# One kernel on one NeuronCore: the running sum of the kept counts and one low part of a weight piece stand behind the first expert's row blocks on VectorE

## The chip, the cores and the metric

The kernel runs on one core of one Trainium2 chip. A core has five engines that run their own instruction streams and wait for each other by semaphores: TensorE (PE; its weight loads are shown as PEld), VectorE (DVE), ScalarE (ACT), GpSimd (POOL) and SyncE (SP, which here only issues DMAs). The metric is the device time of one execution in microseconds, from the first to the last instruction and what lies around them; the median of the runs counts.

## The reference, cut to what matters

Three stages follow each other: a linear attention with a complex decay (its state is a running product, which the kernel computes in chunks), a mixture of experts in which each of 1536 tokens goes to one of 8 experts with room for 384 each, and a bilinear layer.

```python
def _moe_ref(x, w_gate, w1, w2, capacity):
    logits = x @ w_gate
    expert_idx = np.argmax(logits, axis=1)
    ...
    for i in range(N):
        e = expert_idx[i]
        if counts[e] < capacity:
            disp[e, counts[e]] = x[i]
            pos[i] = counts[e]
            counts[e] += 1
            keep[i] = True
    h = np.maximum(np.einsum('ecd,edf->ecf', disp, w1), 0.0)
    y = np.einsum('ecf,efd->ecd', h, w2)
    ...
            out[i] = gate_w[i] * y[expert_idx[i], pos[i]]

def _moe2_ref(x, w_a, w_b, w_out):
    return (x @ w_a) * (x @ w_b) @ w_out
```

The sizes: D = 384, F = 1024, so an expert has NF = 8 column blocks of 128 and KC = 3 row blocks of 128.

## The kernel before, in words

The attention is computed in chunks of 96 tokens for all heads; the gate's logits come out with it, and each chunk's rows are scattered by GpSimd to the place of their expert in a buffer in HBM (`sorted_x`, L795). The last chunks' rows of the first expert don't go through HBM: they are added by matmuls with a 0/1 matrix into three PSUM banks (`rows_bank`, L824). After the last chunk one matmul gives the number of tokens of each expert on all partitions (L979).

Every product with a weight is made exact enough by three matmuls: a value is split into a high part (`..h`, a copy on ACT into the matmul's reduced type) and a low part (`..l`, value minus high part, on DVE). `split` (L1008) issues this pair. For the first expert there are 8 such pieces of w1 (`piece1`, from `queries`, where the first w1 was loaded early), 3 row blocks (`xh`, `xl`, from PSUM) and 8 pieces of w2.

Between the chunks and the experts stands the code that the change touches (L1037 to L1050). DVE clips the counts to the capacity (`kept`, L1039), forms their running sum (`cumk`, L1040) and from it where each expert's first column lies in the output (`fst`, L1041), and casts both to integers (`first`, L1042, `nkept`, L1043). `kept`, `cumk`, `fst` and `one8` are the four slices of one tile, `total`, of 128 x 8 x 4 floats. Then come three weight pieces, the three row blocks and the five other weight pieces.

`nkept` is read by PE (L1117): each expert's matmuls exist for 224 and for 384 columns, and its count picks one. `first` is read by ACT and DVE (L1174, L1175) when they store an expert's outputs at their columns of `yh` and `yl`. POOL clears these two with memsets of 128 x 4608 (L1076) when the last scatter has landed.

`hidden` (L1115) makes the first product of an expert, `outputs` (L1171) the second. In `hidden`, PE takes column blocks f = 0 to 7, each of 9 matmuls (L1129), into four PSUM banks in turn; for the first expert f = 0 and 1 are interleaved by row block. From f = 4 on PE waits until block f - 4 has been read from its bank, that is, for `hl` (L1165) of that block. On ACT and DVE the blocks' `hh` (L1163) and `hl` alternate with w2's pieces. Each engine runs its instructions in the order in which the code issues them. SP loads the next w1 when DVE has made the eighth low part of w1 (L1055). A loop over the six middle experts follows, then the last one, then the bilinear stage in three tiles of 512 tokens.

Of the kernel before, what the change touches and what calls it, by code (L numbers as in the profile page):

```python
# [24 lines left out]
ALU = mybir.AluOpType  # L25
ACT = mybir.ActivationFunctionType
# [42 lines left out]
def build(nc, dims, qk, v, vt, a, w_gate, w1, w2, wa, wb, wo, out, CAP):  # L69
# [12 lines left out]
    KC = DM // P  # L82
    E = w_gate.shape[1]
    F = w1.shape[2]
    NF = F // P
# [14 lines left out]
    def sem(name):  # L100
        return ctx.enter_context(nc.semaphore(name))

    with ctx:
        pe, dve, act, pool = (Queue(nc, n, sem(f"s_{n}")) for n in ("pe", "dve", "act", "pool"))
        sp = nc.sync

        def sb(name, shape, dt=F32, at=ctx, side="left"):
            return at.enter_context(nc.sbuf_tensor(name, shape, dt, side=side))
# [16 lines left out]
        first = sb("first", [P, E], I32)  # L125
        nkept = sb("nkept", [P, E], I32)
# [33 lines left out]
        with att:  # L160
# [83 lines left out]
            vv, ss = nc.vector, nc.scalar  # L244
            tt, stt = vv.tensor_tensor, vv.scalar_tensor_tensor
# [432 lines left out]
            m_oh, m_slot, m_rk, m_tk, m_so, m_hot, m_part_x, m_read_lg = ({} for _ in range(8))  # L678
            s_row0 = sem("s_row0")
            LATE = TAU - 2  # L680
            rows_bank = [bank[i] for i in (2, 3, 6)]
# [300 lines left out]
            kept, cumk, fst, one8 = (total[:, :, i] for i in range(4))  # L982
            pe_chunks, dve_chunks = pe.n, dve.n

            def D_(ins):
                dve.wait(dve.done(ins))
                return (dve, dve.n, False)
# [7 lines left out]
            xh, xl = (sb(n_, [P, KC, CAP], F32R, at=exp_r, side="right") for n_ in ("xh", "xl"))  # L995
# [9 lines left out]
            def z32(x):  # L1005
                return x.bitcast(F32)

            def split(dst_h, dst_l, src):  # L1008

                m = act.done(ss.activation(dst_h, src, ACT.Copy))  # L1010
                dve.wait(m)
                return dve.done(tt(dst_l, src, z32(dst_h), ALU.subtract))  # L1012

            def piece1(f, at_first=False):
                src = raw_0[0].rearrange("p (c f) -> p c f", c=KC) if at_first else raw1
                return [x[:, :, f * P:(f + 1) * P] for x in (w1h, w1l, src)]
# [15 lines left out]
            pe_done, dve_done = (pe, pe_chunks, False), (dve, dve_chunks, False)  # L1032
# [3 lines left out]
            m_w1, m_x0 = [], []  # L1036
            dve.done(vv.memset(one8, 1.0))  # L1037
            dve.wait(m_tl)
            D_(vv.tensor_scalar(kept, rk, float(CAP), None, ALU.min))  # L1039
            D_(vv.tensor_tensor_scan(out=cumk, data0=one8, data1=kept, initial=0.0, op0=ALU.mult, op1=ALU.add))  # L1040
            D_(tt(fst, cumk, kept, ALU.subtract))  # L1041
            dve.done(vv.tensor_copy(first[:], fst))  # L1042
            m_first = dve.done(vv.tensor_copy(nkept[:], kept))  # L1043
            for f in range(NF):
                m_w1.append(split(*piece1(f, True)))
                if f == 2:
                    for c in range(KC):
                        act.wait(m_part_x[c])
                        m_x0.append(split(xh[:, c, :], xl[:, c, :], rows_bank[c][:, 0:CAP]))
                    act.wait(pe_done, dve_done)  # L1050
            sp.wait_ge(pe.sem, pe_chunks)
            sp.wait_ge(dve.sem, dve_chunks)
            sp.wait_ge(s_sc, 16 * TAU)
# [41 lines left out]
            return dve.done(tt(xl[:, :, i * P:(i + 1) * P], s_, z32(xh[:, :, i * P:(i + 1) * P]), ALU.subtract))  # L1095


        pe.wait(m_first)
        PART = 224
        assert PART <= (XT_N - 1) * P  # L1100
        ENG = [mybir.EngineType.PE, mybir.EngineType.DVE, mybir.EngineType.Activation, mybir.EngineType.SP]
# [210 lines left out]
        kept, fst = total[:, :, 0], total[:, :, 2]  # L1312
# [173 lines left out]
```

## Time and profile before

| | us |
|---|---|
| median of 3 runs | 579.62 |
| lowest and highest | 579.06, 599.04 |
| the profiled execution | 581.07 |
| its span, first to last instruction | 579.8 |
| PE busy | 536.5 (93%) |
| DVE busy | 369.1 (64%) |
| ACT busy | 292.6 (50%) |
| POOL busy | 50.8 (9%) |
| mean granted clock of TensorE | 0.969 |

Times in the views are microseconds from the start of the span. A row of the timeline gives start, length, engine, line, operation, what is written and read, and how many instructions of one kind follow each other; the brackets tell how long the engine had stood idle and what released it. Consecutive instructions of one engine overlap a little: a low part of a 128 x 384 piece lasts 0.55 us, while the next starts 0.47 us after it. The matmuls' ends are modelled. A PE busy share of 93% is not PE at its peak.

### The profile page before, as it was taken

What the parts mean: (1) busy time and instruction counts of PE and PEld (TensorE: products, weight loads), DVE (VectorE), ACT (ScalarE), POOL (GpSimd) and SP (SyncE); (2) the same over time, 40 slices, a digit from 0 to 9 for tenths busy, and PEclk for the clock granted to TensorE, in tenths of its full rate; (3) what the DMA queues carried; (4) which work ended last, traced back from release to release, by engine and by line L of the source; (5) the groups of instructions that cost most, each with busy time, mean ns of one, the idle gap of its engine ahead of it and who ended that gap; (6) DMA issues with size and microseconds to landing.
All of it is one profiled execution on the core that took longest, in us unless ns stands there. A gap on an engine that the chain in (4) does not pass through costs nothing.

```text
span 579.8 us, 10188 instructions
## 1 busy us (share of the span) xinstructions
PE 536.5 (93%) x3735; PEld 478.6 (83%) x3736; DVE 369.1 (64%) x900; ACT 292.6 (50%) x681; POOL 50.8 (9%) x63
## 2 busy tenths in 40 slices
PE   0499697889999989999999999999999999999996
PEld 0277365589999989999999998888888888888886
DVE  5998999979889898988888876453321221122121
ACT  5656448656556577878777764443231121311212
POOL 1000000001121233000000000430020000200002
PEclk9967699999999999999999999999999999999999
DMA  8999012589423137656776649720010000100001
GB/s 323 274 388 344 8 54 111 164 230 309 107 63 93 34 112 226 233 191 238 258 252 195 230 137 67 159 83 0 0 55 1 0 1 0 57 0 1 0 1 54
DMA packets 46321, 73.27 MB, mean 126 GB/s; under 512 B 16520, under 2 KB 38792, under 8 KB 45384
## 3 DMA queue, kind: packets, MB, share of 16 engines
q1 hardware_dynamic: 44360, 67.97, 38.5%
q0 software_dynamic: 1920, 4.75, 2.6%
q8 instruction: 27, 0.44, 0.3%
q14 instruction: 14, 0.11, 0.1%
HBM read 55.76 MB, written 16.97 MB: 125 GB/s over the span
## 4 chain that ended last, share of the span: by engine, by line
PE 80%; DVE 9%; ACT 5%; DMA 4%; issue 1%; POOL 0%; SPq 0%; DVEq 0%; POOLq 0%; ACTq 0%
PE psum L1380 26%; PE psum L1353 12%; PE psum L1186 11%; PE psum L1129 11%; PE psum L906 4%; DMA region<-x_rows 3%; PE psum L280 3%; PE psum L707 3%; PE psum L857 3%; PE psum L281 3%; PE psum L908 2%; DVE region L425 2%; PE psum L484 1%; DVE queries L425 1%; DVE region L372 1%
## 5 line engine op out<-in xcount | busy, mean ns | idle before, releaser
L1395 DVE TENSOR_TENSOR ga<-ga,psum 128x512 f32<-128x512 f32 x36 | 24.8, 688 | 128.1 <-PE psum L1380 128.1
L1399 ACT ACTIVATE gh<-ga 128x512 fp32r<-128x512 f32 x36 | 22.8, 632 | 81.8 <-DVE ga L1395 81.8
L1393 ACT ACTIVATE ga<-psum 128x512 f32<-128x512 f32 x36 | 21.5, 598 | 73.1 <-PE psum L1380 73.1
L280 PE MATMUL psum<-region,ident 128*128 128x384 f32 (+1 forms) x42 | 26.5, 725 | 31.8 <-ACT region L290 22.5
L1129 PE MATMUL psum<-xh,w1h 128*128 128x224 f32 x192 | 52.7, 275 | 1.6 <-DVE xl L1012 1.6
L1186 PE MATMUL psum<-hh,w2h 128*128 128x224 f32 x192 | 53.9, 281 | 0.0
L1129 PE MATMUL psum<-xh,w1l 128*128 128x224 f32 x192 | 52.7, 274 | 0.0
L1129 PE MATMUL psum<-xl,w1h 128*128 128x224 f32 x192 | 52.7, 274 | 0.0
L1186 PE MATMUL psum<-hh,w2l 128*128 128x224 f32 x192 | 52.6, 274 | 0.0
L1186 PE MATMUL psum<-hl,w2h 128*128 128x224 f32 x192 | 52.6, 274 | 0.0
L1353 PE MATMUL psum<-woh,gh 128*128 128x384 f32 x144 | 48.3, 335 | 0.4 <-DVE gl L1401 0.4
L1353 PE MATMUL psum<-wol,gh 128*128 128x384 f32 x144 | 48.2, 335 | 0.0
L1353 PE MATMUL psum<-woh,gl 128*128 128x384 f32 x144 | 48.1, 334 | 0.0
L280 PEld LDWEIGHTS psum<-region,ident 128*128 128x128 f32 x42 | 11.0, 281 | 40.6 <-issue 22.2
L1380 PE MATMUL psum<-yh,wah 128*128 128x512 f32 x108 | 42.9, 397 | 0.0
L1380 PE MATMUL psum<-yh,wbh 128*128 128x512 f32 x108 | 42.8, 396 | 0.0
L1380 PE MATMUL psum<-yl,wah 128*128 128x512 f32 x108 | 42.8, 396 | 0.0
L1380 PE MATMUL psum<-yl,wbh 128*128 128x512 f32 x108 | 42.6, 395 | 0.0
L1380 PE MATMUL psum<-yh,wal 128*128 128x512 f32 x108 | 42.6, 395 | 0.0
L1380 PE MATMUL psum<-yh,wbl 128*128 128x512 f32 x108 | 42.6, 395 | 0.0
L1401 DVE TENSOR_TENSOR gl<-ga,gh 128x512 fp32r<-128x512 f32 x36 | 24.9, 693 | 25.2 <-ACT gh L1399 25.2
L1129 PEld LDWEIGHTS psum<-xh,w1h 128*128 128x128 f32 x192 | 36.9, 192 | 1.9 <-DVE xl L1012 1.9
(200 smaller groups left out, 1450.9 us busy)
## 6 DMA issues: line engine op xcount, KB each, us to landing
raw<-w SPq DMA_DIRECT2D x14, 1536.0 KB, 6.6
sorted_x<-region SPq DMA_DIRECT2D x8, 579.0 KB, 14.7
queries<-qk SPq DMA_DIRECT2D x4, 1152.0 KB, 25.5
xrow<-sorted_x SPq DMA_DIRECT2D x7, 579.0 KB, 6.9
region<-x_rows SPq DMA_DIRECT2D x14, 288.0 KB, 3.8
queries<-w SPq DMA_DIRECT2D x2, 1536.0 KB, 15.2
x_rows<-region SPq DMA_DIRECT2D x5, 576.0 KB, 3.3
region<-a SPq DMA_DIRECT2D x2, 1152.0 KB, 8.8
```

Of the source, the lines that this page charges most:

```text
L280: nc.tensor.matmul(x, ident[:], x0[:, cut], start=True, stop=False)
L281: m = nc.tensor.matmul(x, ident[:], x1[:, cut], start=False, stop=True)
L425: m = dve.done(tt(walk(o, [1, 2], [2 * D if n else -2 * D, w], [2, D]), walk(AT_Z[1] + s * W + n * D + i0 * PAIR, [SA, 2], [PAIR, w], [1, D]),
L906: m = nc.tensor.matmul(o, SC[r][:, i, :], with_gate(p), start=True, stop=j == 0)
L1129: m = nc.tensor.matmul(bank[HB0 + f % 4][:, 0:cols], wx[:, c, f * P:(f + 1) * P], xx[:, c, 0:cols], start=c == 0 and i == 0, stop=c == KC ...
L1186: m = nc.tensor.matmul(bank[YB0 + c][:, 0:cols], wx[:, f, c * P:(c + 1) * P], xx[:, f, 0:cols], start=f == 0 and i == 0, stop=f == NF - 1 ...
L1353: m = nc.tensor.matmul(ot[s][:, 0:DM], gx[f % GB3][:, s * P:(s + 1) * P], wx[:, f, :], start=f == 0 and i == 0, stop=f == NF2 - 1 and i == 2)
L1380: m = nc.tensor.matmul(b_[:, 0:TT], wx[:, f, c, :], xx[:, c, t * TT:(t + 1) * TT], start=c == 0 and i == 0, stop=c == KC - 1 and i == 2)
L1393: m = act.done(ss.activation(ga[f % 2][:], ba[:, 0:TT], ACT.Copy))
L1395: m = dve.done(tt(ga[f % 2][:], ga[f % 2][:], bb[:, 0:TT], ALU.mult))
L1399: m = act.done(ss.activation(gh[f % GB3][:], ga[f % 2][:], ACT.Copy))
L1401: m_g.append(dve.done(tt(gl[f % GB3][:], ga[f % 2][:], z32(gh[f % GB3][:]), ALU.subtract)))
```

## The change

`nkept` is cast right after the clipping, straight in front of the first weight piece. After two weight pieces ACT makes the high part of the third, then the row blocks follow, and the low part of the third piece stands behind them on DVE. Behind that come the running sum, the subtraction and the cast to `first`, and then the other five weight pieces. PE waits for `nkept` in place of the last of the casts, and ACT now waits for `first` before its first `hh`. The numbers computed are the same.

```diff
             D_(vv.tensor_scalar(kept, rk, float(CAP), None, ALU.min))
+            m_nkept = dve.done(vv.tensor_copy(nkept[:], kept))
+            for f in range(2):
+                m_w1.append(split(*piece1(f, True)))
+            h_, l_, src = piece1(2, True)
+            m_high = act.done(ss.activation(h_, src, ACT.Copy))
+            for c in range(KC):
+                act.wait(m_part_x[c])
+                m_x0.append(split(xh[:, c, :], xl[:, c, :], rows_bank[c][:, 0:CAP]))
+            dve.wait(m_high)
+            m_w1.append(dve.done(tt(l_, src, z32(h_), ALU.subtract)))
             D_(vv.tensor_tensor_scan(out=cumk, data0=one8, data1=kept, initial=0.0, op0=ALU.mult, op1=ALU.add))
             D_(tt(fst, cumk, kept, ALU.subtract))
-            dve.done(vv.tensor_copy(first[:], fst))
-            m_first = dve.done(vv.tensor_copy(nkept[:], kept))
-            for f in range(NF):
+            m_first = dve.done(vv.tensor_copy(first[:], fst))
+            act.wait(pe_done, dve_done)
+            for f in range(3, NF):
                 m_w1.append(split(*piece1(f, True)))
-                if f == 2:
-                    for c in range(KC):
-                        act.wait(m_part_x[c])
-                        m_x0.append(split(xh[:, c, :], xl[:, c, :], rows_bank[c][:, 0:CAP]))
-                    act.wait(pe_done, dve_done)
...
-        pe.wait(m_first)
+        pe.wait(m_nkept)
+        act.wait(m_first)
```

On VectorE, between the clipping of the counts and the first `hl`, this is the difference of the two orders (`total` is written by the scan, L1040 before and L1050 now, and by the subtraction; `w1l` are the low parts of the weight pieces, `xl` those of the row blocks):

```order
-L1040 SCALAR_TENSOR_TENSOR total<-total 128x8 [waits s_dve]
-L1041 TENSOR_TENSOR total<-total 128x8 [waits s_dve]
-L1042 CAST first<-total 128x8 [waits s_dve]
-L1043 CAST nkept<-total 128x8
-L1012 TENSOR_TENSOR w1l<-queries,w1h 128x3x128 [waits s_act] x3
+L1040 CAST nkept<-total 128x8 [waits s_dve]
+L1012 TENSOR_TENSOR w1l<-queries,w1h 128x3x128 [waits s_act] x2
 L1012 TENSOR_TENSOR xl<-psum,xh 128x384 [waits s_act] x3
+L1049 TENSOR_TENSOR w1l<-queries,w1h 128x3x128
+L1050 SCALAR_TENSOR_TENSOR total<-total 128x8
+L1051 TENSOR_TENSOR total<-total 128x8 [waits s_dve]
+L1052 CAST first<-total 128x8 [waits s_dve]
```

Only the cast to `nkept` and two weight pieces are left ahead of the row blocks; the third piece, the scan, the subtraction and the cast to `first` stand behind them.

On ScalarE, from the first weight piece to the first `hh`, before:

```order
L1010 ACTIVATE w1h<-queries 128x3x128 [waits s_w1]
L1010 ACTIVATE w1h<-queries 128x3x128 x2
L1010 ACTIVATE xh<-psum 128x384 [waits s_pe] x3
L1010 ACTIVATE w1h<-queries 128x3x128 [waits s_dve]
L1010 ACTIVATE w1h<-queries 128x3x128 x4
L1163 ACTIVATE hh<-psum 128x384 [waits s_w2,s_pe]
```

and the same place of the changed kernel:

```order
L1010 ACTIVATE w1h<-queries 128x3x128 [waits s_w1]
L1010 ACTIVATE w1h<-queries 128x3x128
L1044 ACTIVATE w1h<-queries 128x3x128
L1010 ACTIVATE xh<-psum 128x384 [waits s_pe] x3
L1010 ACTIVATE w1h<-queries 128x3x128 [waits s_dve]
L1010 ACTIVATE w1h<-queries 128x3x128 x4
L1169 ACTIVATE hh<-psum 128x384 [waits s_w2,s_dve,s_pe]
```

Nothing moved on ScalarE; its first `hh` has a wait for VectorE more, the one for `first`. PE's, POOL's and SP's instructions keep their order.

## Rows read from the trace of the kernel before

**Rows 1.** Busy time by stretch: stretch, its length, each engine's busy time, clock, DMA
```profile
225.00:345.00 120.00, 120.00 (x1077) 119.89 (x1076) 101.13 (x214) 90.35 (x212) 0.00 (x0) 1.00 0.63 216
```

**Rows 2.** Chain that ended last: start, length, what
```profile
213.96 8.27 PE psum L1129 x72
```

**Rows 3.** Timeline of VectorE, from the scan to the first hl
```profile
211.28 0.18 DVE L1040 TENSOR_TENSOR_SCAN total<-total 128x8 f32<-128x8 f32 x1
...
211.78 0.17 DVE L1043 CAST nkept<-total 128x8 int32<-128x8 f32 x1
211.85 1.49 DVE L1012 TENSOR_TENSOR w1l<-queries,w1h 128x384 fp32r<-128x384 f32 x3
213.26 1.48 DVE L1012 TENSOR_TENSOR xl<-psum,xh 128x384 fp32r<-128x384 f32 x3
214.65 2.42 DVE L1012 TENSOR_TENSOR w1l<-queries,w1h 128x384 fp32r<-128x384 f32 x5
216.99 0.55 DVE L1165 SCALAR_TENSOR_TENSOR hl<-psum,hh 128x384 fp32r<-128x384 f32 x1
```

**Rows 4.** Timeline of TensorE: first matmul of f = 0 and of f = 4
```profile
213.96 0.34 PE L1129 MATMUL psum<-xh,w1h 128*128 128x224 f32 x1 [1.57 <-DVE xl L1012]
...
218.04 0.27 PE L1129 MATMUL psum<-xh,w1h 128*128 128x224 f32 x1
```

**Rows 5.** Timeline of ScalarE: the row blocks, and the next expert's first pieces
```profile
211.73 1.25 ACT L1010 ACTIVATE xh<-psum 128x384 fp32r<-128x384 f32 x3 [0.73 <-PE psum L824]
...
223.61 0.94 ACT L1010 ACTIVATE w1h<-raw 128x384 fp32r<-128x384 f32 x2 [0.45 <-DMA raw<-w]
```

**Rows 6.** Timeline of GpSimd: the memsets of yh and yl
```profile
214.24 3.96 POOL L1076 MEMSET yh<- 128x4608 f32 x1
218.14 3.95 POOL L1076 MEMSET yl<- 128x4608 f32 x1
```

**Rows 7.** Timeline: GpSimd's scatters and VectorE's L745 beside them
```profile
135.22 1.09 POOL L795 DMA_INDIRECT sorted_x<-region,sloti  x1 [12.70 <-DVE route L737]
...
135.68 0.23 DVE L745 TENSOR_SCALAR ohb<-route 96x8 bf16<-96x8 f32 x1
...
145.94 0.92 POOL L795 DMA_INDIRECT sorted_x<-region,sloti  x1 [4.64 <-DVE route L734]
...
146.54 0.29 DVE L745 TENSOR_SCALAR ohb<-route 96x8 bf16<-96x8 f32 x1
...
167.30 0.92 POOL L795 DMA_INDIRECT sorted_x<-region,sloti  x1 [3.33 <-DVE route L734]
...
167.86 0.33 DVE L745 TENSOR_SCALAR ohb<-route 96x8 bf16<-96x8 f32 x1
168.23 0.47 POOL L939 IOTA region<- 96x384 f32 x1
```

**Rows 8.** L745: count, shortest, median and longest ns, first and last start
```profile
L745 DVE TENSOR_SCALAR ohb<-route x16: 227/287/328, 130.8 to 209.4; 96x8 bf16<-96x8 f32 x16
```

**Rows 9.** L248, a cast of 96 elements, columns as in rows 8
```profile
L248 DVE CAST trib<-tri x1: 205/205/205, 3.4 to 3.4; 96x96 bf16<-96x96 f32 x1
```

**Rows 10.** Timeline of SyncE's queue: the load of the next w1
```profile
217.10 0.37 SPq L1023 DMA_DIRECT2D raw<-w  x1
```

**Rows 11.** Stretches of 1 us around TensorE's pauses, columns as in rows 1
```profile
63.00:64.00 1.00, 0.28 (x1) 0.00 (x0) 1.00 (x3) 0.68 (x1) 0.00 (x0) 1.00 0.00 0
...
65.00:66.00 1.00, 0.00 (x0) 0.00 (x0) 1.00 (x6) 1.00 (x2) 0.00 (x0) 0.79 0.00 0
...
72.00:73.00 1.00, 1.00 (x4) 0.53 (x3) 1.00 (x4) 0.00 (x0) 0.00 (x0) 0.79 0.00 0
...
96.00:97.00 1.00, 0.83 (x8) 0.49 (x5) 1.00 (x6) 1.00 (x4) 0.00 (x0) 1.00 0.00 0
...
99.00:100.00 1.00, 0.00 (x0) 0.00 (x0) 1.00 (x2) 1.00 (x2) 0.00 (x0) 0.86 0.00 0
...
103.00:104.00 1.00, 1.00 (x4) 0.58 (x4) 1.00 (x6) 0.00 (x0) 0.00 (x0) 0.94 0.73 160
```

## The prediction

> **What bounds the kernel now.** I read four views: the mean clock and busy time in stretches, the chain that ended last, the timeline of each engine from 208 to 226 us, and the lines that a few shapes stand on. From 225 to 345 us PE is busy for all of its 120 us at full clock [rows 1]; the chain that ended last runs through PE there, from its first expert's 72 matmuls on [rows 2]. So whatever moves PE around 214 us moves the end by as much. The edit lies in the one place before it where the chain is VectorE's: PE's first expert starts at 213.96, 1.57 us after its last matmul, released by the low part of the first row block [rows 4]. From 211.28 on DVE works without a gap: the sum of counts, the subtraction and two casts (211.28 to 211.85), three weight pieces, three row blocks, five weight pieces, and at 216.99 the first `hl` [rows 3].
>
> **What the edit takes off in front of PE.** Between the clipping of the counts and the first weight piece only the cast to `nkept` is left. In the rows, scan start to first piece is 0.57 us, and `nkept` to first piece 0.07 [rows 3]. Now `nkept` starts where the scan did, at 211.28, and the first piece at 211.35: 0.50 us less. One piece fewer stands ahead of the row blocks: three starts take 1.41 us (211.85 to 213.26), so one is 0.47. The first row block starts at 213.26 - 0.97 = 212.29. ACT's part of it began at 211.73 with three in 1.25 us, so about 0.49 each, and is there at 212.22 [rows 5]: just in time. From the row block's start to PE's first matmul it is 0.70 us now [rows 3, 4]. PE would start at 212.99, **0.97 us earlier**.
>
> **Why that isn't the gain.** Nothing leaves DVE's queue: the same instructions stand ahead of the first `hl`, in another order. PE's fifth column block (f = 4) writes the bank that `hl` of block 0 must have read, 36 matmuls after the first. Before, that was due at 218.04 [rows 4], and `hl` was ready at 216.99 + 0.55 = 217.54, so it cost nothing. Now PE gets there at 212.99 + 4.08 = 217.07. Row blocks at 212.29, 212.76, 213.23, third piece at 213.70, scan at 214.17, subtraction and cast behind it: the small three take 0.50 (from the same rows), so the fourth piece starts at 214.67 where it was 214.65, and `hl` at 217.01. It ends at 217.56; by the 0.15 us between a row block's end (213.26 + 0.55) and its matmul, PE goes on at 217.71. If this were all, the sum would be 218.04 - 217.71 = **0.33 us faster**. Later blocks are due every 1.02 us (9 matmuls) while `hl` comes every 0.93 (two steps), so no second stall follows.
>
> **What the cast to `first` now stands beside.** It stood between the scan and the cast to `nkept`, before 211.78 and so before POOL's big memsets. It moves to about 214.58, and POOL fills `yh` from 214.24 for 3.96 us, then `yl` from 218.14 for 3.95 [rows 6]; nothing in the edit moves them, as they wait for the last scatter. The weight and row pieces (two inputs) run beside these memsets at their 0.55 us, so those are not hurt. But the trace shows that a DVE instruction with one SBUF input and an SBUF output is held by a POOL instruction: L745 (96 x 8, float in, bf16 out) takes 0.23 us alone or early beside a scatter (135.68, POOL began 0.46 before), and 0.29 to 0.33 where it starts 0.56 to 0.60 us into one [rows 7, 8]. There its end is tied to POOL's: 146.54 + 0.29 = 146.83 against 145.94 + 0.92 = 146.86; 167.86 + 0.33 = 168.19 against 168.22. Twelve of the sixteen show this, each ending 0.03 to 0.04 us before POOL; the other four have no scatter beside them or start 0.2 to 0.5 us into it. That is a hold until POOL lets go. The `first` cast is of that kind (128 x 8, one input, both sides in SBUF). The cast at L248 needs 205 ns for 96 elements [rows 9], where the two-input form needs about 1 ns an element (0.55 us for 384, and 0.17 for a cast of 8 [rows 3]), so some 260: such casts move more than one element at a time, which fits their using a second way into memory that POOL shares.
>
> What the rows price is a hold of at most 0.33 - 0.23 = 0.10 us, beside a scatter; none shows such a cast beside a memset. So the bounds of this cost are: nothing; 0.1 us; up to the end of the first memset (218.20); up to the end of the second (222.09). I take the first memset's end: a memset writes all the time, as the scatter seems to do only in its last part, and the tie to POOL's end is the same mechanism.
>
> The Trainium skill, SBUF — State Buffer, section Who interferes with whom, says that VectorE in a two-port mode and GpSimd exclude each other for a whole instruction, first come first served, and that copies and casts can enter that mode; two-input instructions collide only with a GpSimd instruction that reads. That the two-input pieces beside the memset keep their 0.55 us agrees; a whole-memset hold isn't shown in this trace. By the page the sum would be that of the next paragraph, by the longest hold in the rows alone 0.33 - 0.10 = 0.23 us faster.
>
> **The sum with the hold.** The cast ends 0.03 before POOL's end, at 218.17, and the next piece starts 0.10 before a cast's end (211.78 + 0.17 against 211.85 [rows 3]): the fourth piece at 218.07 instead of 214.65, 3.42 us later. Behind it in DVE's queue stand four more pieces and `hl`, which moves from 216.99 to 220.41, ends at 220.96, and lets PE's f = 4 start at 221.11. Against 218.04 that is **3.07 us slower**. PE pauses twice: before f = 3 (about 216.2 to 218.77, for the fourth piece) and before f = 4. ACT waits for the same cast ahead of its first `hh`, but its queue catches up inside this. The load of the next w1 waits for DVE's eighth piece and goes out at 220.5 in place of 217.10; it took 6.5 us until ACT began at 223.61 [rows 5, 10], so 227.1, and DVE isn't free for it before 227.9 (220.41 and 16 steps of 0.47). From there DVE is 3.4 us later than before and PE 3.1; the 0.3 between them hides in DVE's idle time, 18.9 us of the 120 from 225 on [rows 1]. Without that cover it would be added.
>
> **Clock.** After PE stopped at 63.28 the granted clock fell from full to half (2.4 to 1.2 GHz) at about 65.6, 2.3 us later, and was back at 72.4; after the stop at 96.83 it fell at about 99.7, 2.9 us later, and was back at 103.1 [rows 11]. (Where within a slice it changed follows from the slice's mean: 0.79 is 0.58 us at full clock.) The pause before f = 3 is 2.6 us, between the two. If the clock falls, that is at 218.5 to 219.1, and by the two stretches of 6.8 and 3.4 us it is back at 221.9 to 225.9; PE loses half of the time since 221.1, so 0.4 to 2.4. If it doesn't, 0. I take 0.4, from the shorter stretch, since the pause in front of it is the nearer in length. Sum: 3.07 + 0.4 = **3.5 us slower**. The profiled execution took 581.07 (span 579.8), 1.45 above the median of the runs shown; I set the difference against the median: 579.62 + 3.5 = **583.1**.
>
> **Rivals.**
> 1. The cast isn't held (or by 0.1 us only): 0.23 to 0.33 us faster, 579.3. For it: no row has a cast beside a memset; eight elements are few. Against it: the twelve tied ends. It also comes if DVE reaches the cast before POOL's memset, which takes 0.34 us of lead. The place is the one cast; the decision lies at a hold of 0.33 us. Chance 0.28.
> 2. POOL doesn't let go between its memsets: they overlap by 0.06 us [rows 6]. The cast would end at 222.06, f = 4 start 3.89 us later still: 6.96 slower, and up to 2.4 for the clock, whose fall is then near certain: 586.6 to 589.0. Against it: held instructions end before POOL's own end, so the way is open before the second one starts; L745 at 167.86 slips out although an IOTA follows its scatter after 0.01 us [rows 7]. Chance 0.12.
> 3. No change at all, 579.6: PE's start is held by something else, such as ACT's row block coming 0.07 us before it is wanted, and the fifth block by `hl` a third of a microsecond late for another reason. Chance 0.05.
> 4. Something dearer, with PE or a load thrown out of step for longer, over 591: it would take a hold of 12 us, three memsets long. Chance 0.03.
>
> **Numbers.** The forecast has 0.52, its own range is 582.3 to 585.3. Executions scatter by about half a microsecond. For 8 in 10 the range takes in rival 1 and 3: 578.8 to 586.0, which leaves out rival 2, rival 4 and a little of the scatter. Two per cent is 11.6 us, about what a measurement of this kernel can tell from no change: only rival 4 and the far end of rival 2 reach it. Faster by over 2% 0.01, within 0.95, slower by over 2% 0.04.
>
> **What would show it.** The `first` cast at about 214.6: 0.17 us long (rival 1), about 3.6 us (forecast), 7.5 (rival 2). PE's first expert starts at 213.0 in all of them. PE's wait before f = 3: none, 2.6 or 6.5 us; before f = 4: 0.6, 1.3, 1.3. The fourth weight piece at 214.67, 218.07 or 221.96. The memsets stay at 214.2. If the first matmul isn't about 1 us earlier, the first part is wrong; if the cast is short, the hold is wrong and the sign with it.

## The result, and the profile after

| | before | changed |
|---|---|---|
| median of 6 runs, us | 579.54 | 587.79 |
| lowest to highest, us | 579.06 to 599.04 | 586.09 to 588.71 |
| the profiled execution, us | 581.07 | 587.91 |
| its span, us | 579.8 | 586.6 |
| mean granted clock | 0.969 | 0.964 |

The 599.04 us of the kernel before is an execution in a slow state, which the ratio leaves out. The ratio of the runs is 1.0132, with a 95% interval of 1.0111 to 1.0154: the changed kernel is 6.4 to 8.9 us slower. That is within 2%, but above the forecast of 583.1 and above the end of its range, 586.0. The direction was right, and the size was that of rival 2.

The two executions were not equally fast ahead of the edit: the clipping of the counts stands at 211.09 before and at 209.46 after. So places are compared below by their distance from the clipping ("+5.95" is 5.95 us after it).

VectorE's timeline in the changed kernel, from the clipping to the first `hl` (it answers to [rows 3]):

```profile
209.46 0.15 DVE L1039 TENSOR_SCALAR total<-psum 128x8 f32<-128x8 f32 x1
...
209.65 0.17 DVE L1040 CAST nkept<-total 128x8 int32<-128x8 f32 x1
209.73 1.02 DVE L1012 TENSOR_TENSOR w1l<-queries,w1h 128x384 fp32r<-128x384 f32 x2
210.67 1.48 DVE L1012 TENSOR_TENSOR xl<-psum,xh 128x384 fp32r<-128x384 f32 x3
212.06 0.55 DVE L1049 TENSOR_TENSOR w1l<-queries,w1h 128x384 fp32r<-128x384 f32 x1
...
212.74 0.18 DVE L1051 TENSOR_TENSOR total<-total 128x8 f32<-128x8 f32 x1
212.95 7.90 DVE L1052 CAST first<-total 128x8 int32<-128x8 f32 x1
213.03 7.82 DVE L1012 TENSOR_TENSOR w1l<-queries,w1h 128x384 fp32r<-128x384 f32 x5
221.46 0.56 DVE L1171 SCALAR_TENSOR_TENSOR hl<-psum,hh 128x384 fp32r<-128x384 f32 x1 [0.60 <-ACT hh L1169]
```

Up to the subtraction everything is as the prediction worked it out. Then the cast of eight numbers lasts 7.90 us, to 220.85. The row under it is to be read closely: five weight pieces start behind the cast at their usual step, and end with it. GpSimd's timeline of the same stretch (it answers to [rows 6]):

```profile
209.80 1.28 POOL L795 DMA_INDIRECT sorted_x<-region,sloti  x1 [1.29 <-DVE total L1039]
212.86 0.12 POOL L1077 MEMSET tag<- 128x24 f32 x1 [1.78 <-DMA sorted_x<-region,sloti]
212.93 0.14 POOL L1078 IOTA at_row<- 128x12 f32 x1
213.01 3.94 POOL L1081 MEMSET yh<- 128x4608 f32 x1
216.89 3.93 POOL L1081 MEMSET yl<- 128x4608 f32 x1
```

The last memset ends at 220.82, and the cast 0.03 us behind it. The cast began 0.06 us before the memset of `yh`, inside the IOTA in front of it, and wasn't let through at that IOTA's end, nor at 216.95 between the two memsets. TensorE's timeline (it answers to [rows 4]): the start of f = 0, the last matmul of f = 2, the start of f = 3.

```profile
211.37 0.34 PE L1135 MATMUL psum<-xh,w1h 128*128 128x224 f32 x1 [0.60 <-DVE xl L1012]
...
214.34 0.27 PE L1135 MATMUL psum<-xh,w1l 128*128 128x224 f32 x1
220.93 0.56 PE L1135 MATMUL psum<-xh,w1h 128*128 128x224 f32 x1 [6.32 <-DVE w1l L1012]
```

The first matmul now waits 0.60 us where it waited 1.57 [rows 4], and stands at +1.91 instead of +2.87: 0.96 us earlier. Then PE stands still for 6.32 us. The stretches around this pause (stretch, length, each engine's busy time, granted clock, DMA share, GB/s; they answer to [rows 11]):

```profile
216.00:217.00 1.00, 0.00 (x0) 0.00 (x0) 1.00 (x6) 0.00 (x0) 1.00 (x2) 0.98 0.21 74
217.00:218.00 1.00, 0.00 (x0) 0.00 (x0) 1.00 (x6) 0.00 (x0) 1.00 (x1) 0.50 0.00 0
...
227.00:228.00 1.00, 1.00 (x10) 1.00 (x9) 0.41 (x1) 0.90 (x2) 0.00 (x0) 0.90 0.12 33
```

The granted clock fell from full to half (2.4 to 1.2 GHz) at about 216.96 and was back at about 227.2. PE worked at half clock from 220.93 on, about 6.3 us. The chain that ended last (start, length, what) shows both losses, and answers to [rows 2]:

```profile
212.95 7.90 DVE first L1052
220.85 0.08 DVE w1l L1012 x5
220.93 8.26 PE psum L1135 x45
```

The 45 matmuls are those of f = 3 to 7. From the start of f = 3 to the first matmul of the second product it is 8.10 us (+11.47 to +19.57), and before it was 5.07 (+5.95 to +11.02); the clock cost 3.03. **The whole account:** f = 3 comes 5.52 later than before, the clock adds 3.03, and the second product is 8.55 later. From the second product to the end of the span both traces take the same, 357.7 us before and 357.6 after, so the 8.55 reaches the end as it is. The medians differ by 8.25, and nothing else is needed to explain the time. The load of the next w1 left SP late, as a result of the same hold, and nobody waited for it further on (it answers to [rows 10]):

```profile
220.99 0.37 SPq L1023 DMA_DIRECT2D raw<-w  x1
```

### The profile page after: what moved, and what is told of

Same layout as the page of the kernel before. It is cut to its first block, busy times and chain, and to the rows that moved or that the text cites. A ratio compares the mean times of both kernels' runs of the same rounds, so it can differ in the third digit from the quotient of the medians.

```text
span 586.6 us, 10188 instructions
## 1 busy us (share of the span) xinstructions
PE 537.2 (92%) x3735; PEld 479.6 (82%) x3736; DVE 374.8 (64%) x900; ACT 292.6 (50%) x681; POOL 51.3 (9%) x63
## 4 chain that ended last, share of the span: by engine, by line
PE 77%; DVE 12%; ACT 5%; DMA 4%; issue 1%; POOL 0%; SPq 0%; DVEq 0%; POOLq 0%; ACTq 0%
PE psum L1386 26%; PE psum L1359 12%; PE psum L1135 11%; PE psum L1192 11%; PE psum L906 3%; DMA region<-x_rows 3%; PE psum L707 3%; PE psum L857 3%; PE psum L280 3%; PE psum L281 2%; PE psum L908 2%; DVE region L425 2%; DVE queries L425 1%; DVE first L1052 1%; DVE region L372 1%
## 5 line engine op out<-in xcount | busy, mean ns | idle before, releaser
L1135 PE MATMUL psum<-xh,w1h 128*128 128x224 f32 x192 | 54.3, 283 | 6.9 <-DVE w1l L1012 6.3
L1135 PE MATMUL psum<-xl,w1h 128*128 128x224 f32 x192 | 54.0, 281 | 0.0
L1135 PE MATMUL psum<-xh,w1l 128*128 128x224 f32 x192 | 54.0, 281 | 0.0
L1135 PEld LDWEIGHTS psum<-xh,w1h 128*128 128x128 f32 x192 | 38.2, 199 | 7.4 <-DVE w1l L1012 6.5
```

What stands on the lines that cost most here:

```text
L1135: m = nc.tensor.matmul(bank[HB0 + f % 4][:, 0:cols], wx[:, c, f * P:(f + 1) * P], xx[:, c, 0:cols], start=c == 0 and i == 0, stop=c == KC ...
```

## The experiments

Places after the clipping, in us, and the cast or copy that each kernel puts beside the memsets. "Second product" is its first matmul. Four kernels were run once, e3, e4, e6 and e9; what is read from them is read from the places in their traces, and their times are only set beside it.

| kernel | cast | f = 0 | f = 3 | f = 4 | second product | median (runs), us |
|---|---|---|---|---|---|---|
| before | none there | 2.87 | 5.95 | 6.95 | 11.02 | 579.5 |
| changed | 7.90 | 1.91 | 11.47 | 13.53 | 19.57 | 587.79 (6) |
| e1 two inputs | 0.17 | 1.91 | 4.99 | 6.62 | 11.04 | 578.67 (10) |
| e2 POOL later | 0.17 | 1.91 | 4.99 | 6.61 | 10.98 | 578.45 (10) |
| e3 gap | 4.01 | 1.91 | 7.59 | 8.82 | 13.23 | 580.31 (1) |
| e4 six memsets | 8.03 | 1.91 | 11.60 | 13.67 | 19.39 | 586.68 (1) |
| e5 cast added | 6.98 | 2.87 | 5.95 | 11.28 | 17.00 | 585.63 (4) |
| e6 probes | 7.58 | 1.90 | 11.44 | 13.50 | 18.06 | 586.21 (1) |
| e7 piece only | none there | 2.40 | 5.48 | 6.60 | 10.95 | 578.69 (8) |
| e8 sums later | none there | 1.91 | 4.99 | 6.11 | 10.77 | 578.56 (12) |
| e9 sum only | 7.89 | 2.38 | 11.46 | 13.52 | 19.64 | 587.92 (1) |

**The same value by an instruction with two inputs.** This leaves the order of every engine alone and changes only the kind of the one instruction.

```diff
-            m_first = dve.done(vv.tensor_copy(first[:], fst))
+            m_first = dve.done(tt(first[:], cumk, kept, ALU.subtract))
```

> The integer starts in `first` come from a two-input subtraction on VectorE instead of a one-input cast of `fst`; same place, same order. Theory A (a one-input instruction between SBUF and SBUF is held by GpSimd's memsets, a two-input one is not): the instruction takes 0.2 us in place of 7.90, no pause before the fourth column block, the fifth waits about 0.6 us for `hl`; from the start of the clipping of the counts to the first matmul of the second product 10.7 us (11.02 before, 19.73 changed); time 0.3 us under the kernel before, so about 579.3, ratio 0.999. Theory B (the place itself is bad, for instance anything behind the scan waits for the memsets, or the memsets hold all of VectorE): still about 7.9 us long, 587 us.

VectorE's timeline of this kernel, the same place:

```profile
215.03 0.17 DVE L1052 TENSOR_TENSOR first<-total 128x8 int32<-128x8 f32 x1
215.12 2.43 DVE L1012 TENSOR_TENSOR w1l<-queries,w1h 128x384 fp32r<-128x384 f32 x5
```

and GpSimd's:

```profile
214.99 0.14 POOL L1078 IOTA at_row<- 128x12 f32 x1
215.07 3.95 POOL L1081 MEMSET yh<- 128x4608 f32 x1
```

In the same place beside the IOTA, 0.04 us before the memset, the instruction takes 0.17 us, the pieces behind it 2.43. The whole loss is gone: the ratio to the kernel before is 0.999 (0.9971 to 1.0008). ScalarE still waits for `first` here, so that new wait alone costs nothing that shows.

**The cast kept, GpSimd later.** Here the cast is untouched, and the memsets wait for it.

```diff
-        pool.wait(pe_done, dve_done)
+        pool.wait(pe_done, dve_done, m_first)
```

> The changed kernel, with GpSimd waiting for `first` before its memsets of tag, yh and yl. Theory A: the cast has nothing beside it, 0.17 us long; memsets start right after it, about 0.3 us later than they would; 10.7 us from clipping to the second product, ratio 0.999 to the kernel before. Theory B (the cast is slow for its operands or its place, whoever runs on GpSimd): still 7.9 us long and 587 us.

The two engines' timelines of this kernel:

```profile
212.34 0.17 DVE L1052 CAST first<-total 128x8 int32<-128x8 f32 x1
```

```profile
212.62 0.12 POOL L1077 MEMSET tag<- 128x24 f32 x1 [2.15 <-DVE first L1052]
```

The very cast that took 7.90 us takes 0.17 ahead of GpSimd's work; the ratio is 0.9993 (0.9971 to 1.0015). So the loss needs both: this kind of instruction, and GpSimd at work. Either one taken away is enough. The expectation had the second product at 10.7 in both kernels; it came at 11.04 and 10.98, which is taken up further down.

**Why two memsets and not one.** The prediction had the cast slip out at the end of the first. In this kernel GpSimd waits for its own first memset before it starts the second.

```diff
             m_y0 = pool.done(g.memset(z32(x[:, :, 0:N]), 0.0))
+            pool.wait(m_y0)
```

> The changed kernel, with GpSimd waiting for its own semaphore between the memset of yh and that of yl. Theory A1 (GpSimd doesn't give way between two instructions that follow without a wait, but does when it waits): the cast ends at the end of the yh memset, about 4.0 us long, the second memset starts after it; the pause of TensorE before the fourth block is about 2.5 us instead of 6.3 and the clock may stay up; stage from clipping to second product 14.0 to 16 us. Theory A2 (GpSimd always wins the next turn too): 7.9 us as before. Theory A3 (whoever waits longest goes next, and only the overlap of the two memsets kept the cast out) gives the same as A1.

VectorE's and GpSimd's timelines, and TensorE's at f = 3:

```profile
211.65 4.01 DVE L1052 CAST first<-total 128x8 int32<-128x8 f32 x1
```

```profile
211.70 3.94 POOL L1081 MEMSET yh<- 128x4608 f32 x1
215.70 3.95 POOL L1081 MEMSET yl<- 128x4608 f32 x1
```

```profile
215.75 0.37 PE L1136 MATMUL psum<-xh,w1h 128*128 128x224 f32 x1 [2.43 <-DVE w1l L1012]
```

One wait, and the cast ends at 215.66, with the first memset. The memsets now stand 0.06 us apart, where they overlapped by 0.06. This is the case that the prediction took for the likeliest, and its pause before f = 3 (2.6 forecast, 2.43 measured) is right for it. The clock stayed at 1.00 in every stretch from 213 to 219. The second product stands at 13.23, under the 14.0 to 16 expected; the time of this one run, 580.31, is less far above the kernel before (579.63) than these 2.2 us, because its clipping came early, at 208.16.

**More boundaries without a wait.** Each memset is cut into three of a third, with no wait between them.

```diff
-            m_y0 = pool.done(g.memset(z32(x[:, :, 0:N]), 0.0))
+            for c in range(KC):
+                m_y0 = pool.done(g.memset(z32(x[:, c, 0:N]), 0.0))
```

> The changed kernel, with each of GpSimd's two big memsets cut into three of a third (six in a row, no wait between them). Theory A1 (GpSimd keeps the way open to itself as long as its next instruction follows without a wait; a wait of its own let the cast through at 4.0 us): the cast is again 7.9 us long although six ends of memsets lie in between, and the stage from the clipping of the counts to the first matmul of the second product takes 17 to 20 us. Theory A3 (the cast gets through at some end of an instruction, with the overlap of the two long ones an exception): 1.3 to 5 us long, stage 11 to 15 us.

```profile
212.06 4.01 POOL L1082 MEMSET yh<- 128x1536 f32 x3
216.02 4.02 POOL L1082 MEMSET yl<- 128x1536 f32 x3
```

Five boundaries, and the cast lasts 8.03 us, over all six (212.03 to 220.06 in its row on VectorE; the last memset ends at 220.04). So it isn't the length of one instruction that sets the hold, but how long GpSimd has instructions one right behind the other. What let go was a wait of GpSimd that left 0.06 us between two instructions. Each boundary over which the cast was held is one at which GpSimd's instructions overlap by 0.05 to 0.06 us; whether a boundary with neither overlap nor wait would hold it stays open, and so does whether the gap or the wait itself lets go.

**The mechanism in the kernel before.** Nothing is moved here; one cast of the same kind is added after the fourth weight piece, into a tile that nobody reads.

```diff
                 m_w1.append(split(*piece1(f, True)))
+                if f == 3:
+                    dve.done(vv.tensor_copy(spare[:], fst))
```

> The kernel before, its order untouched, with one more cast of 128 x 8 from `fst` to a spare tile behind the fourth weight piece, where GpSimd's memsets run. Theory A: this cast alone is held until the end of the yl memset (7 us or so, from about 215.1 to 222.1 in that kernel's time), the later weight pieces end with it, TensorE pauses before its fifth block for about 4 us, and the time is 5 to 8 us over the kernel before (ratio 1.009 to 1.014). Theory B (the loss comes from what the change did to the order or from ScalarE's new wait, not from the cast's neighbour): the cast takes 0.17 us and the ratio is 1.000.

VectorE's timeline of this kernel:

```profile
212.03 6.98 DVE L1048 CAST spare<-total 128x8 int32<-128x8 f32 x1
212.11 6.91 DVE L1013 TENSOR_TENSOR w1l<-queries,w1h 128x384 fp32r<-128x384 f32 x4
213.99 5.03 DVE L1168 SCALAR_TENSOR_TENSOR hl<-psum,hh 128x384 fp32r<-128x384 f32 x1
214.45 4.57 DVE L1013 TENSOR_TENSOR w2l<-queries,w2h 128x384 fp32r<-128x384 f32 x1
214.92 4.10 DVE L1168 SCALAR_TENSOR_TENSOR hl<-psum,hh 128x384 fp32r<-128x384 f32 x1
```

A cast that has nothing to do with the edit costs 6.0 us (585.63 against 579.63; ratio 1.0116, 1.0099 to 1.0133). Seven instructions start behind it at their step of 0.47 and all end at 219.02, GpSimd's last memset having ended at 218.99. PE had all weight pieces for f = 3 and stops at f = 4 instead, whose weight piece and `hl` are both among the seven:

```profile
219.28 0.34 PE L1132 MATMUL psum<-xh,w1h 128*128 128x224 f32 x1 [4.16 <-DVE hl L1168]
```

and the granted clock falls around its return:

```profile
219.00:220.00 1.00, 0.72 (x5) 0.75 (x6) 0.98 (x11) 0.00 (x0) 0.00 (x0) 0.82 0.00 0
...
223.00:224.00 1.00, 1.00 (x11) 1.00 (x10) 0.33 (x1) 0.85 (x2) 0.00 (x0) 0.97 1.01 418
```

At half from about 219.6 to 223.0, half of 3.4 us: 1.7 (the 36 matmuls from f = 4 to the second product take 5.72 instead of 4.07). The wait moved f = 4 by 4.33 (11.28 - 6.95); 4.33 + 1.65 = 5.98, close to the 6.0 between the medians. So the second instance gives the same account as the first, with other sizes. It is less exact here: in this trace the stretch from the second product to the end is 0.8 us longer than before (358.5 against 357.7). That part arises little by little in the bilinear stage, over 130 us behind the hold, and its cause is open.

**Which instructions are held.** The kernel with two inputs, and behind `first` four small probes into a spare tile: a copy out of PSUM, a reduction of 8 elements, a copy of one element, a copy of four.

```diff
+            dve.done(vv.tensor_copy(spare[:, 0:2], rows_bank[2][:, 0:2]))
+            dve.done(vv.tensor_reduce(out=spare[:, 2:3], in_=kept, axis=AXX, op=ALU.add))
+            dve.done(vv.tensor_copy(spare[:, 3:4], kept[:, 0:1]))
+            dve.done(vv.tensor_copy(spare[:, 4:8], kept[:, 0:4]))
```

> The kernel with `first` from a two-input subtraction, and four small probes into a spare tile right behind it, beside the yh memset: a copy of 2 elements from PSUM, a sum over 8 elements in SBUF, a copy of 1 element in SBUF, a copy of 4 elements in SBUF, in this order (they add work and change no output). Theory A (only copies and casts with both ends in SBUF that move two elements at a time are held): the first three 0.15 to 0.2 us, the last about 7.5 us. If one element is held too, the third is already 7.5 us long. Theory C (every one-input instruction is held): the first is.

```profile
212.31 0.15 DVE L1054 COPY spare<-psum 128x2 f32<-128x2 f32 x1
212.38 0.15 DVE L1055 TENSOR_REDUCE spare<-total 128x1 f32<-128x8 f32 x1
212.45 0.14 DVE L1056 COPY spare<-total 128x1 f32<-128x1 f32 x1
212.51 7.58 DVE L1057 COPY spare<-total 128x4 f32<-128x4 f32 x1
```

The memset of `yh` began at 212.26, before all four. Three pass beside it in 0.15 us, and the copy of four elements waits to the end of `yl` at 220.07. What was held has one input with both sides in SBUF, and more than one element; the cast isn't what matters, nor are eight elements needed. Each probe ran once, so the line between one and four elements isn't drawn closer than that.

**The halves of the edit alone.** First only the third piece's low part behind the row blocks, with both casts in their old place:

```diff
-            for f in range(NF):
+            for f in range(2):
                 m_w1.append(split(*piece1(f, True)))
...
+            dve.wait(m_high)
+            m_w1.append(dve.done(tt(l_, src, z32(h_), ALU.subtract)))
+            act.wait(pe_done, dve_done)
+            for f in range(3, NF):
```

> The kernel before with one half of the change alone: the low part of the third weight piece stands behind the row blocks; scan, subtraction and both casts stay where they were, ahead of the memsets. No cast is held. TensorE starts 0.47 us earlier relative to the clipping (2.40 us after it, 2.87 before), the fifth block is due at 6.48 and `hl` lets it go at 6.60 (6.95 before). If the gain stays, the second product starts at 10.7 (11.02 before); if TensorE's sequencer has lost its lead over the engine by the wait and the branch to the second product costs it back, as in the two runs without a hold (11.04 and 10.98), at 11.0. Time within 0.1% of the kernel before either way.

Then only the running sum behind the row blocks, with three pieces ahead of them:

```diff
-            for f in range(2):
+            for f in range(3):
                 m_w1.append(split(*piece1(f, True)))
-            h_, l_, src = piece1(2, True)
-            m_high = act.done(ss.activation(h_, src, ACT.Copy))
...
-            dve.wait(m_high)
-            m_w1.append(dve.done(tt(l_, src, z32(h_), ALU.subtract)))
```

> Only the running sum's half of the change: the cast to nkept alone ahead, all three weight pieces ahead of the row blocks, then the scan, the subtraction and the cast to first. Theory (the hold is all, and it needs only that the cast starts within POOL's run of IOTA and two memsets): the same instructions stand ahead of the cast as in the changed kernel, so it starts 3.5 us after the clipping and is held for 7.9 us to the end of the second memset; f = 3 starts at 11.5 us after the clipping, the second product near 19.7, and the time is 586 to 589, though PE begins its first expert at 2.4 instead of 1.91 us. Rival (both halves are needed, since only the third piece's low part behind the row blocks, alone harmless, brings the cast into the memset): the cast takes 0.17 us and the time is 578 to 580.

The piece alone: first matmul 0.47 us earlier, ratio 1.0001 (0.9968 to 1.0033), no gain and no loss. The sum alone, on VectorE and GpSimd:

```profile
212.75 7.89 DVE L1048 CAST first<-total 128x8 int32<-128x8 f32 x1
```

```profile
212.72 0.14 POOL L1074 IOTA at_row<- 128x12 f32 x1
212.81 3.94 POOL L1077 MEMSET yh<- 128x4608 f32 x1
```

Again the cast starts inside the IOTA, before the memset. The second product stands at +19.64, where the full edit has it at +19.57, and the one run took 587.92. The third piece's move isn't needed for the loss.

**Can the idea be made to pay?** The sums go further back: the scan behind the first `hl`, and the subtraction and `first`, in the form with two inputs, behind the second. The order on VectorE, in words, is `nkept`, two pieces, row blocks, six pieces, `hl`, scan, piece, `hl`, subtraction, `first`.

```diff
-            m_first = dve.done(vv.tensor_copy(first[:], fst))
...
-        act.wait(m_first)
...
+                if at_first and f == 1:
+                    dve.wait(m_sum)
+                    dve.done(tt(fst, cumk, kept, ALU.subtract))
+                    first_mark.append(dve.done(tt(first[:], cumk, kept, ALU.subtract)))
...
+        act.wait(first_mark[0])
```

> Meant to beat both: `nkept` first and the third piece's low part behind the row blocks as in the change, but the scan stands behind the first `hl`, the subtraction behind the second, and `first` comes from a second two-input subtraction; ScalarE waits for `first` only before it reads it. Theory: VectorE has 0.5 us less ahead of the first `hl`, so it is ready about 6.1 us after the clipping; TensorE, at its fifth block from 6.0 on, waits 0.1 at most; second product at 10.2 to 10.5 (11.02 before). Then a loss of 0.2 or so is possible at the turning of the second row tile, which waits for VectorE. Time 0.4 to 0.8 us under the kernel before (ratio 0.9986 to 0.9993). Rival: VectorE's load per expert decides, and the gain is gone by the next expert: 0.0 us.

f = 4 comes 0.84 us earlier than before (+6.11 against +6.95). The second product comes only 0.25 earlier, at 10.77 where 10.2 to 10.5 was expected, and waits now for something else, as TensorE's timeline shows:

```profile
219.26 0.37 PE L1197 MATMUL psum<-hh,w2h 128*128 128x224 f32 x1 [0.37 <-DVE w2l L1012]
```

VectorE's queue holds the same work, so most of what PE gains in front it gives back where it next needs VectorE. The rest isn't lost later: from the second product to the end it is 357.7 us in both traces, so the rival's 0.0 us isn't borne out, but a quarter of a microsecond is too little for the runs to tell. The ratio is 0.9992 (0.9976 to 1.0007): no version here beats the kernel before by an amount that these runs can tell.

## Why the prediction missed

**Where PE starts: right.** 0.96 us earlier against 0.97 worked out.

**That the cast is held, and by what: right.** The kernel with two inputs and the one with late memsets show it from two sides. That the tie between L745's ends and the scatters' ends [rows 7, 8] is the same mechanism fits them, but no run tests it. The Trainium skill, SBUF — State Buffer, section Who interferes with whom, states the exclusion of the two engines and that casts can fall under it; that the cast is held agrees with it, and so does the two-input form's 0.17 us beside an IOTA and a memset; the length of the hold, 7.90 us, doesn't.

**How long: the step that failed.** "I take the first memset's end" gave a delay of 3.42 us and a cast of about 3.6, where the hold went on to the second's end: the cast lasted 7.90. The reason against it, in rival 2, was that "the way is open before the second one starts". It rested on L745 at 167.86, which ended 0.04 us before the IOTA behind the scatter began [rows 7]. That was the wrong witness: behind its scatter the IOTA began 0.01 us after the end, so there was a gap, though a small one, while the second memset begins 0.06 us before the first one ends [rows 6]. The row that mattered was, as far as these runs show, that overlap; that it was the 0.01 us of gap that let L745 out, and not that a scatter is another kind of instruction, isn't shown. The kernels with a wait (4.01) and with six memsets (8.03) decide it. The forecast's number for one memset was close; the mis-sized term was the count of memsets. In the sum, the 3.07 for the hold should have been 5.52 (taken at f = 3), and the 0.4 for the clock, which such a long pause then lowered, 3.03: the two make up the 5.1 us between the forecast difference and the measured one. Rival 2 should have had the larger chance.

**What waits behind the cast: wrong, in the kernel's favour.** The prediction let VectorE stand still and start the fourth piece 0.10 us before the cast's end, with four pieces and `hl` still to do. In fact the instructions behind run on and only end with the held one. "Its queue catches up inside this" wasn't right for ScalarE either: in the kernel with the gap its first `hh`, which waits for `first`, starts at 215.75, 0.09 us after the cast's end, the first `hl` ends at 216.83, and f = 4 starts 0.15 behind it, 0.23 later than its own nine matmuls would have let it. That kernel shows the size: f = 4 at +8.82, so 1.87 later than before, where the forecast had 3.07; its second product is 2.21 later. By that mistake rival 2's 6.96 us was too high for the wait: measured are 5.52 at f = 3, the last place before PE's work at half clock adds to it.

**The clock: right in kind, too small.** Rival 2 was given "up to 2.4", the forecast's own upper bound (half of 221.1 to 225.9) carried over; from rival 2's own restart of PE at 222.66 (its fourth piece at 221.96, and 0.70) the same end gives 1.6. It goes back to the 6.8 us stretch in [rows 11], and that wasn't the longest in this trace. In the kernel before, the granted clock was also at half from about 38.3 to 48.5, for 10.2 us, with PE at work throughout (columns as in rows 11):

```profile
38.00:39.00 1.00, 1.00 (x10) 1.00 (x10) 1.00 (x5) 0.97 (x2) 0.00 (x0) 0.64 1.07 366
...
48.00:49.00 1.00, 1.00 (x4) 0.52 (x3) 1.00 (x4) 0.00 (x0) 0.00 (x0) 0.74 0.97 306
```

In the changed kernel it stayed at half for 10.2 us too, and cost 3.0. A pause of 2.43 us (e3) didn't lower it, one of 4.16 lowered it for 3.4 us, those of 6.32, of 6.45 (e4) and of 5.84 (e9) cost 3.0, 2.7 and 3.1. It isn't a matter of the pause's length alone: in e6, with a pause of 6.3, the clock was at half for 6.9 us only (216.54 to 223.4) and cost 1.55 (6.62 from f = 3 to the second product, against 5.07). What ends the low stretch earlier there stays open. The forecast's 0.4 for its own case would have been 0. The two errors in rival 2, 1.4 too much and 0.6 too little, partly cancel: that its 586.6 to 589.0 holds the result is in part luck.

**The margin before the memset: wrong, without effect on the size.** The prediction had the memset start 0.34 us before the cast; it started 0.06 after it. Nearly all of that is the scatter: 1.28 us instead of 0.92. In all kernels where the first weight piece starts 0.27 us after the clipping (changed, e1 to e4, e6, e8, e9) the scatter takes 1.27 or 1.28; in those where it starts 0.77 after it (before, e5, e7) it takes 0.92. The scatter starts 0.34 after the clipping, so in the first group it finds a two-input piece already running. That such a piece slows it is argued from this order in eleven kernels, and wasn't tried by itself. The cast was caught all the same, by the small instructions that GpSimd runs in front of the big memset: the memset of `tag` had begun 0.09 us before it, the IOTA 0.02. So rival 1's condition, the cast reached before the memset, did come about, and wasn't enough.

**The gain without a hold: 0.33 forecast, about none found.** f = 4 does come 0.33 us earlier in e1 (6.62 against 6.95), but the second product doesn't (11.04 against 11.02). From f = 4 to it are 36 matmuls: 4.07 us before, 4.37 in e2. TensorE's timeline of e2, f = 4 and the entry to the second product:

```profile
215.46 0.34 PE L1135 MATMUL psum<-xh,w1h 128*128 128x224 f32 x1 [0.45 <-DVE hl L1171]
215.64 0.28 PE L1135 MATMUL psum<-xl,w1h 128*128 128x224 f32 x1
...
219.44 0.27 PE L1135 MATMUL psum<-xh,w1l 128*128 128x224 f32 x1
219.83 0.37 PE L1192 MATMUL psum<-hh,w2h 128*128 128x224 f32 x1
```

and the second of these places in the kernel before:

```profile
221.95 0.28 PE L1129 MATMUL psum<-xh,w1l 128*128 128x224 f32 x1
222.11 0.36 PE L1186 MATMUL psum<-hh,w2h 128*128 128x224 f32 x1
```

The first step after a stop is 0.18 us instead of 0.11 (0.07 lost), and the step over the branch to the second product is 0.39 instead of 0.16 (0.23 lost): together the 0.30. At that branch PE reads `nkept` again, and its sequencer comes there with less lead after a stop. That reading of the 0.23 is an inference from the times; the 0.30 itself is shown. Rival 1's case was therefore one of no change.

## What to carry to other kernels

Before a small copy or cast is moved on VectorE, look at what GpSimd does at the new place, and take the price from the whole unbroken run of its instructions, not from the one that is running. An instruction with two inputs for the same value (here a subtraction into the integer tile), or a wait that lets the cast go first, took the hold away here and cost nothing that shows. For the two-input form this is shown beside an IOTA and memsets, and beside nothing else. When a stall is moved towards TensorE, ask of its length also whether the clock will fall: a wait of 2.4 us cost itself, one of 4.2 us 1.7 more, waits of 5.8 to 6.5 us 1.5 to 3.1 more.

## What the runs showed of the hardware

- GpSimd keeps a waiting VectorE copy out over instructions that follow each other without a gap (each starts 0.05 to 0.06 us before the one ahead of it ends): 7.90 us over an IOTA and two memsets, 8.03 over an IOTA and six memsets, 4.01 where it waits for itself after the first. The Trainium skill, SBUF — State Buffer, section Who interferes with whom, speaks of one whole instruction. By that rule the hold would have ended with the IOTA during which the cast began, or at 216.95, with the first memset, and the measurement decides against both.
- While it is held, the instructions behind it start at their usual step, five to seven of them, and all are reported done only when it is (220.85 in the changed kernel, 219.02 in e5). Such a row of instructions with one common end marks a hold in a timeline. Their mean durations in the groups of the profile say nothing of their work.
- Held was a copy of four elements (7.58 us) and casts of eight; not held were a copy of one element, one of two elements out of PSUM, a reduction, and the two-input subtraction (0.14 to 0.17).
- The granted clock fell about 2.4 us after PE's last matmul in the changed kernel (214.61 to 216.96), and about 4.5 us after it in e5 (215.12 to 219.6), just after PE had started again. How long it then stayed low, 10.2 and 3.4 us, differed as well, and after equal pauses of 6.3 us it was 10.2 and, in e6, 6.9. A stretch of 10.2 at half also stands in the kernel before (38.3 to 48.5), through which PE worked.
